# A fused attention and mixture-of-experts kernel: weight pieces split elsewhere in the opening, unused products in TensorE's waits, record scatters issued later

## The chip, the core and the metric

The kernel runs on one core of a Trainium2 chip. The metric is the device time of one execution in microseconds. Before the change three timed runs gave 1045.49, 1046.57 and 1046.40 us, median 1046.4. One further execution was profiled; its own time is 1038.92 us, and its span from first to last instruction is 1037.2 us.

## The reference

Three layers in a row over 4608 tokens (8 batches of 576), model width 512, hidden width 1024:

```python
# attention, in chunks of 64 tokens, 8 heads of 64
scores = scale * np.matmul(q_c, k_c.transpose(0, 1, 2, 4, 3))
attn = softmax(scores)
out = np.matmul(attn, v_c)                      # -> x, (4608, 512)
# first feed-forward layer
h = x @ w_in                                    # (4608, 1024)
solu = h * softmax(h)
ln = (solu - mean) / np.sqrt(var + 1e-06) * g_ln
x2 = ln @ w_out                                 # (4608, 512)
# mixture of 8 experts: one expert for each token
e_idx = np.argmax(x2 @ w_gate, axis=1)
out[mask] = gate_w[mask, None] * eom[mask, e, None] * (relu(x2[mask] @ w1[e]) @ w2[e])
```

The gain `g_ln` is a factor of each row of `w_out`, and the kernel multiplies it into the weights.

## The kernel before

The work is in units of 128 tokens, 36 of them. Every large product is made from fp32 values split in a rounded high part and a remainder (the low part), as three products: high by high, high by low weight, low by high weight. So every weight must be split too: the high part by a copy that rounds, the low part by a subtraction of source minus high part.

Each engine has its own instruction order, written out by hand as steps `s` from -2 to 35; engines wait for each other by semaphores. In step `s` unit `s` is in its first-layer products (`H_ps`, 24 products of 128x512, L458), unit `s - 1` in its second-layer products (`Y_ps`, 24 products), unit `s + 1` has its probabilities transposed (L475) and multiplied by v (`mixed`, L534 to L547), and unit `s + 2` has its scores made (`scores`, L521 to L532). "H(0)" below is the first-layer products of unit 0, "Y(0)" the second-layer products of unit 0.

The path of one unit: TensorE makes scores; VectorE takes the maximum and subtracts it (L948, L951); ScalarE takes the exponential in place (L767); VectorE sums, adds 1e-9 (L957), inverts and multiplies (L962, semaphore `norm`); TensorE transposes the result; ScalarE copies it to SBUF (`pT`, L703); TensorE multiplies by v; ScalarE makes the high part `xh` (L703), VectorE the low part `xl` (L899); then H. VectorE takes the maximum of a row of H (L922), ScalarE the exponential (L747), VectorE multiplies (L930) and subtracts the mean (L937); TensorE transposes the rows, ScalarE makes `dh`, VectorE `dl`; then Y. GpSimd makes the factor of each row (`xs_ops`), and ScalarE applies it when it copies Y out (L776).

The opening, steps -2 to 1, has another job beside this: 4 MB of first-layer weights, in 8 pieces of 128x1024. Pieces 0 to 3 are `w_in`, pieces 4 to 7 `w_out`. SyncE's queue loads a piece into one of four staging places (`HOME`); ScalarE makes its high part at the places of its program that `HIGH_PIECES` names (L716 to L728); for pieces 4 to 7 it first multiplies both halves by `g_ln`, in place. The low part is made by VectorE for pieces 1 to 3 (`LOW_PIECES`, L901 to L905), by GpSimd for 0 and 4 to 7 (L1242 to L1245). Between pieces 0 and 4 GpSimd issues nine DMAs that fill a table (L1297 to L1300). Step 0 of SyncE then loads the first expert's weights over two of the staging places, and GpSimd splits those.

Later, once in four units, the routing of four units is worked out, and GpSimd scatters their records to the table by four indirect DMAs (`send`, L1288 to L1294), as soon as VectorE has them. The second phase (the experts) begins when the last unit is through; nothing of it is touched.

## Time and profile before

| | |
|---|---|
| median of three runs | 1046.4 us |
| profiled execution, its own time | 1038.92 us |
| its span | 1037.2 us |
| TensorE busy | 1011.7 us (98%) |
| VectorE, ScalarE, GpSimd busy | 545.9, 403.0, 259.7 us |
| share of TensorE in the chain that ended last | 92% |
| 0 to 36.4 us: TensorE busy | 20.59 us |

How the rows further down are read. A row of the timeline gives start (us from the span's start), duration (us), engine, line and operation, output and input, xcount of merged instructions, and in brackets the idle time of the engine before it and what ended that. A row of the chain of waits gives start, duration and what. A row of a stretch gives its length, then busy time and count for TensorE, its weight loads, VectorE, ScalarE and GpSimd, then the granted clock, the busy share of the DMA engines and GB/s. Starts of neighbouring matmuls overlap a little, since each one's end is modelled.

### The profile page before, as it was taken

To read this page: it belongs to the slowest core of one execution; us is meant where nothing else is said; L and a number is where in the kernel's file an instruction comes from. 1 tells how busy PE (TensorE), PEld (TensorE's weight loads), DVE (VectorE), ACT (ScalarE), POOL (GpSimd) and SP (SyncE) were. 2 spreads that over 40 slices of the span, in tenths; PEclk is the share of its full clock that TensorE was granted. 3 is DMA by queue.
4 is the path that set the end of the run, shared out by engine and by line. 5 is a ranking of instruction groups with operands and counts; after the bars stand their busy time and mean duration, and the time that the engine had idled before them with its cause. 6 is when DMAs were issued, how large, how long until landed. Compare 5 with 4: busy or idle time off the path is not lost.

```text
span 1037.2 us, 24250 instructions
## 1 busy us (share of the span) xinstructions
PE 1011.7 (98%) x7323; PEld 837.9 (81%) x7324; DVE 545.9 (53%) x1137; ACT 403.0 (39%) x733; POOL 259.7 (25%) x458
## 2 busy tenths in 40 slices
PE   5899999999999999999999999999999999999997
PEld 4788888888888888888878788888888888888885
DVE  5676767677666767676737534244243332342521
ACT  5544434444334444344422533233333432342521
POOL 5772202113031312122223222122222221122211
PEclk9999999999999999999999999999999999999999
DMA  8452332322122322222013444334232331341110
GB/s 294 158 163 82 48 81 78 82 82 73 61 72 82 82 75 53 78 82 62 22 52 102 173 133 160 122 94 122 90 122 91 112 122 50 100 127 55 34 41 30
DMA packets 43024, 97.15 MB, mean 94 GB/s; under 512 B 9678, under 2 KB 9806, under 8 KB 42960
## 3 DMA queue, kind: packets, MB, share of 16 engines
q1 hardware_dynamic: 31616, 75.51, 23.6%
q0 software_dynamic: 9248, 20.70, 6.3%
q8 instruction: 46, 0.75, 0.3%
q10 hardware_dynamic: 2096, 0.04, 0.1%
q14 instruction: 18, 0.15, 0.0%
HBM read 76.66 MB, written 20.60 MB: 94 GB/s over the span
## 4 chain that ended last, share of the span: by engine, by line
PE 92%; DMA 3%; issue 1%; ACT 1%; SPq 1%; DVE 1%; POOL 0%; POOLq 0%; DVEq 0%; ACTq 0%
PE Y_ps L442 38%; PE H_ps L442 38%; PE X L434 7%; PE S L434 3%; PE S L530 2%; PE X L544 2%; DMA stage<-in_experts 1%; PE L_ps L518 1%; DMA stage<-in_moe_w_in 1%; PE L_ps L442 1%; SPq L391 0%; DMA xg<-x_rows,slot_rec 0%; POOL route_table L1293 0%; DVE dl L899 0%; ACT stage L726 0%
## 5 line engine op out<-in xcount | busy, mean ns | idle before, releaser
L442 PE MATMUL Y_ps<-wx,dh 128*128 128x512 f32 (+1 forms) x1184 | 376.3, 399 | 1.3 <-DVE dl L899 1.3
L442 PE MATMUL H_ps<-wx,xh 128*128 128x512 f32 (+1 forms) x1216 | 334.4, 397 | 2.9 <-DVE xl L899 2.3
L442 PEld LDWEIGHTS H_ps<-wx,xh 128*128 128x128 f32 x1216 | 223.4, 189 | 46.1 <-issue 2.4
L442 PEld LDWEIGHTS Y_ps<-wx,dh 128*128 128x128 f32 x1184 | 214.1, 188 | 43.9 <-DVE dl L899 1.4
L442 PE MATMUL Y_ps<-wx,dl 128*128 128x512 f32 (+1 forms) x592 | 231.8, 391 | 0.0
L442 PE MATMUL H_ps<-wx,xl 128*128 128x512 f32 (+1 forms) x608 | 187.9, 390 | 0.0
L899 DVE TENSOR_TENSOR dl<-X,dh 128x512 fp32r<-128x512 f32 x152 | 97.6, 684 | 80.8 <-ACT dh L703 80.8
L899 DVE TENSOR_TENSOR wx<-stage,wx (+1 forms) x58 | 70.5, 1225 | 122.0 <-ACT wx L865 119.4
L442 PEld LDWEIGHTS H_ps<-wx,xl 128*128 128x128 f32 x608 | 114.4, 188 | 24.5
L442 PEld LDWEIGHTS Y_ps<-wx,dl 128*128 128x128 f32 x592 | 111.1, 188 | 24.4
L922 DVE TENSOR_REDUCE nmax_h<-H_ps 128x1 f32<-128x1024 f32 x36 | 44.1, 1224 | 85.3 <-PE H_ps L442 85.3
L703 ACT ACTIVATE stage<-S 128x512 f32<-128x512 f32 x36 | 21.5, 598 | 170.9 <-PE S L434 170.9
L703 ACT ACTIVATE dh<-X 128x512 fp32r<-128x512 f32 x152 | 81.7, 592 | 7.4 <-DVE i_load L1184 4.4
L1251 POOL TENSOR_TENSOR var<-sumsq 128x1 f32<-128x1 f32 x36 | 7.0, 193 | 300.3 <-ACT stage L761 300.3
L803 ACT ACTIVATE cen<-H_ps 128x512 f32<-128x512 f32 x40 | 23.9, 597 | 145.5 <-PE H_ps L442 145.5
L434 PE MATMUL X<-ident,cen 128*128 128x128 f32 x608 | 78.8, 272 | 0.2 <-ACT cen L803 0.2
L434 PEld LDWEIGHTS X<-ident,cen 128*128 128x128 f32 x608 | 70.7, 140 | 10.2 <-ACT cen L803 0.3
L865 ACT ACTIVATE wx<-stage x56 | 58.6, 1058 | 44.7 <-issue 23.2
L1339 POOL DMA_INDIRECT out<-x,slot_rec x40 | 41.9, 1047 | 134.5 <-ACT x L829 121.9
L829 ACT ACTIVATE x<-Y_ps,slot_rec 128x512 f32<-128x512 f32 x39 | 26.8, 687 | 115.8 <-PE Y_ps L442 115.8
L1069 DVE TENSOR_SCALAR cen<-H_ps 128x512 f32<-128x512 f32 x40 | 27.6, 690 | 78.5 <-PE H_ps L442 78.5
L930 DVE SCALAR_TENSOR_TENSOR cen<-H_ps,cen 128x1024 f32<-128x1024 f32 x36 | 44.1, 1225 | 30.2 <-ACT cen L747 30.2
(199 smaller groups left out, 1026.0 us busy)
## 6 DMA issues: line engine op xcount, KB each, us to landing
stage<-in_experts SPq DMA_DIRECT2D x64, 512.0 KB, 3.5
stage<-in_q SPq DMA_DIRECT2D x36, 256.0 KB, 3.1
stage<-in_k SPq DMA_DIRECT2D x36, 256.0 KB, 3.8
stage<-in_v SPq DMA_DIRECT2D x36, 256.0 KB, 3.6
x_rows<-x SPq DMA_DIRECT2D x36, 256.0 KB, 2.0
stage<-in_moe_w_out SPq DMA_DIRECT2D x4, 512.0 KB, 5.2
stage<-in_moe_w_in SPq DMA_DIRECT2D x3, 512.0 KB, 7.1
slot_rec<-route_table POOLq DMA_DIRECT2D x40, 2.0 KB, 2.7
```

The costliest lines, as they stand in the source:

```text
L434: last = pe.transpose(to[:, i * n:(i + 1) * n], x, idn)
L442: i = pe.matmul(acc[:, c0:c0 + HALF], x[:, kk, :], w(part, kk * cols + c0), start=first and x is hi and part == 0, stop=last and x is lo)
L530: i = pe.matmul((S_ps, T0)[a][e * CH:(e + 1) * CH, r * CH:(r + 1) * CH], qT[b][rows, 2 * r + e, :], kT[b][rows, 2 * r + e, :], start=True, ...
L703: act.activation(out_, in_, ACT.Copy).then_inc(done, 1)
L803: act.activation(hs[:, 0:HALF], H_ps[:, 0:HALF], ACT.Relu).then_inc(h0_ev, 1)
L829: act.activation(yb[(u + 1) % 2][:, :], Y_ps[:, :] if has(0) else H_ps[:, 0:DM], ACT.Copy, scale=slot_rec[(u + 3) % 4][:, 2:3].bitcast(f32 ...
L865: act.activation(hi, src, ACT.Copy).then_inc(split_hi, 1)
L899: dve.tensor_tensor(out_, whole, high.bitcast(f32), ALU.subtract).then_inc(done, 1)
L922: dve.tensor_reduce(nmax_h[:, 0:1], H_ps[:, :], AX.X, ALU.max, negate=True).then_inc(hmax, 1)
L930: dve.scalar_tensor_tensor(cen[:, :], H_ps[:, :], 1.0, cen[:, :], ALU.mult, ALU.mult, accum_out=sum_t[:, 0:1]).then_inc(he_done, 1)
L1069: dve.tensor_scalar(hs[:, HALF:], H_ps[:, HALF:], 0.0, None, ALU.max).then_inc(h1_ev, 1)
L1339: pool.indirect_dma_start(out, bass.IndirectOffsetOnAxis(ap=slot_rec[(u + 3) % 4][:, 1:2].bitcast(u32), axis=0), yb[(u + 1) % 2][:, :], No ...
```

## The change

- Piece 4 gets a fifth staging place and is loaded behind the first two units' rows, without a wait. Pieces 5, 6 and 7 move to other places and wait for other pieces. Pieces 6 and 7 are issued ahead of unit 3's q and k.
- ScalarE makes the high part of piece 3 one step later, behind the copy `pT` of unit 0 (the place "prob").
- Pieces 5 and 7 are no longer scaled in place: ScalarE scales and rounds in one instruction per half, and VectorE makes the low part as source times gain minus high part, one instruction per half: piece 5 behind the maximum of H(0), piece 7 behind unit 2's subtraction.
- GpSimd makes the low part of piece 0 in two halves, the second behind `norm` of unit 0; that of piece 4 between the table's fifth and sixth DMA; that of piece 6 behind them.
- TensorE makes 20 products into `Y_ps` that nothing reads (`warm`), at six places of steps -2 to 0.
- A chunk's four scatters wait for `pv_done` of the next step, that is for the products with v of the next step.

```diff
...
 
-        staged = [x[:, :].rearrange("p (l n) -> p l n", l=2) for x in (spare, cen)] + [raw[:, b, :, :] for b in range(2)]
-        HIGH_PIECES = {(-2, "begin"): (0,), (-2, "exp"): (1, 2, 3), (-1, "x"): (4,), (-1, "exp"): (5,), (0, "x"): (6, 7)}
-        LOW_PIECES = {(-2, "norm"): (1,), (-1, "x"): (2, 3)}
+        staged = [x[:, :].rearrange("p (l n) -> p l n", l=2) for x in (spare, cen)] + [raw[:, b, :, :] for b in range(2)] + [stage[:, 0:4:3, 1, :]]
+        HIGH_PIECES = {(-2, "begin"): (0,), (-2, "exp"): (1, 2), (-1, "prob"): (3,), (-1, "x"): (4,), (-1, "exp"): (5,), (0, "x"): (6, 7)}
+        LOW_PIECES = {(-2, "norm"): (1,), (-1, "x"): (2, 3), (0, "max"): (5,), (0, "exp"): (7,)}
+        ACT_SCALED = (4, 6)
 
-        HOME = (0, 1, 2, 3, 0, 2, 3, 0)
-        USE = (0, 0, 0, 0, 1, 1, 1, 2)
+        HOME = (0, 1, 2, 3, 4, 0, 2, 3)
+        USE = (0, 0, 0, 0, 0, 1, 1, 1)
 
...
                 else:
-                    free, count = {4: (wlow_pool, 1), 5: (wlow_dve, 2), 6: (wlow_dve, 3), 7: (wlow_pool, 2)}[i]
-                    sp.wait_ge(free, count)
+                    if i > KD:
+                        sp.wait_ge(*{5: (wlow_pool, 1), 6: (wlow_dve, 2), 7: (wlow_dve, 3)}[i])
                     rows = w_out[(i - KD) * 2 * P:(i - KD + 1) * 2 * P, :]
...
             load_v(0, 1, 1)
+            load_first(KD)
             sp.wait_ge(qk_done, 1)
             load_qk(0, 2, 0)
-            for i in range(KD, KD + 2):
-                load_first(i)
+            load_first(KD + 1)
 
...
                 s = c * UN + u
-                if has(4) and not (isinstance(s, int) and s == -2):
-                    sp.wait_ge(qk_done, s + 3)
-                    load_qk(c + 1, u, u % 2)
                 if isinstance(s, int) and s == -1:
...
                         load_first(i)
+                if has(4) and not (isinstance(s, int) and s == -2):
+                    sp.wait_ge(qk_done, s + 3)
+                    load_qk(c + 1, u, u % 2)
                 if has(3) and not (isinstance(s, int) and s == -2):
...
                 if isinstance(s, int) and s == 0:
-                    sp.wait_ge(wlow_pool, 5)
+                    sp.wait_ge(wlow_pool, 3)
+                    sp.wait_ge(wlow_dve, 5)
                     for p in range(2):
...
 
+            def warm(count):
+
+                hi = first_at(0, 0)
+                for _ in range(count):
+                    pe.matmul(Y_ps[:, :], hi[:, 0, 0:P], hi[:, 1, :], start=True, stop=True)
+
             def step(c, u, has):
...
                     transposed(T1, [x2[u % 2][:, kk * P:(kk + 1) * P] for kk in range(KD)], ident[:, :]).then_inc(x2_tp, 1)
+                if isinstance(s, int) and s == 0:
+                    warm(2)
                 if has(1):
...
                     transposed(T0, [prob[:, 2 * r:2 * r + 2, :].rearrange("p a c -> p (a c)") for r in range(4)], ident[:, :]).then_inc(pt_tp, 1)
+                if isinstance(s, int) and s in (-1, 0):
+                    warm(s + 2)
                 if has(-1):
...
                     scores(c, u, b)
+                if isinstance(s, int) and s == -2:
+                    pe.wait_ge(wsplit_hi, 1)
+                    warm(6)
+                if isinstance(s, int) and s == -1:
+                    warm(3)
                 if has(1) and not (isinstance(s, int) and s == -1):
                     mixed(c, u, has)
+                if isinstance(s, int) and s == 0:
+                    warm(6)
                 if has(-1):
...
                 if isinstance(s, int) and s == 1 and kk % 2 == 0:
-                    pe.wait_ge(wlow_pool, kk // 2 + 2)
+                    low, count = ((wlow_pool, 2), (wlow_dve, 4), (wlow_pool, 3), (wlow_dve, 5))[kk // 2]
+                    pe.wait_ge(low, count)
 
...
                         f = (i - KD) * 2
-                        for l in range(2):
-                            act.activation(staged[HOME[i]][:, l, :], staged[HOME[i]][:, l, :], ACT.Copy, scale=gl[:, f + l:f + l + 1]).then_inc(wscaled, 1)
-                        act.wait_ge(wscaled, (i - KD + 1) * 2)
-                        act.activation(first_at(0, i), staged[HOME[i]], ACT.Copy).then_inc(wsplit_hi, 1)
+                        if i in ACT_SCALED:
+                            for l in range(2):
+                                act.activation(staged[HOME[i]][:, l, :], staged[HOME[i]][:, l, :], ACT.Copy, scale=gl[:, f + l:f + l + 1]).then_inc(wscaled, 1)
+                            act.wait_ge(wscaled, ACT_SCALED.index(i) * 2 + 2)
+                            act.activation(first_at(0, i), staged[HOME[i]], ACT.Copy).then_inc(wsplit_hi, 1)
+                        else:
+                            act.activation(first_at(0, i)[:, 0, :], staged[HOME[i]][:, 0, :], ACT.Copy, scale=gl[:, f:f + 1])
+                            act.activation(first_at(0, i)[:, 1, :], staged[HOME[i]][:, 1, :], ACT.Copy, scale=gl[:, f + 1:f + 2]).then_inc(wsplit_hi, 1)
 
...
                     copy(pT[:, :, :], quad(T0, H), pt_ev)
+                first_high(s, "prob")
                 if has(0):
...
                     dve.wait_ge(wsplit_hi, i + 1)
-                    less(first_at(1, i), staged[HOME[i]], first_at(0, i), wlow_dve)
+                    if i < KD:
+                        less(first_at(1, i), staged[HOME[i]], first_at(0, i), wlow_dve)
+                    else:
+                        lo, x, hi, f = first_at(1, i), staged[HOME[i]], first_at(0, i).bitcast(f32), (i - KD) * 2
+                        dve.wait_ge(gl_in, 48)
+                        dve.scalar_tensor_tensor(lo[:, 0, :], x[:, 0, :], gl[:, f:f + 1], hi[:, 0, :], ALU.mult, ALU.subtract)
+                        dve.scalar_tensor_tensor(lo[:, 1, :], x[:, 1, :], gl[:, f + 1:f + 2], hi[:, 1, :], ALU.mult, ALU.subtract).then_inc(wlow_dve, 1)
 
...
                     dve.tensor_reduce(nmax_h[:, 0:1], H_ps[:, :], AX.X, ALU.max, negate=True).then_inc(hmax, 1)
+                first_low(s, "max")
                 if has(-2):
...
                                       smax[:, :].rearrange("p (r a) -> p r a", a=2).unsqueeze(3).to_broadcast([P, H // 2, 2, CH]), ALU.subtract).then_inc(ssub, 1)
+                    first_low(s, "exp")
                     dve.wait_ge(exp_s, s + 3)
...
 
+            def first_low_half(i, l):
+
+                return pool.tensor_tensor(first_at(1, i)[:, l, :], staged[HOME[i]][:, l, :], first_at(0, i)[:, l, :].bitcast(f32), ALU.subtract)
+
             def xs_ops(s):
...
                 if u == 2 and has(-2) and not (isinstance(c, int) and c == 0):
+
+                    wait_alone(pool, pv_done, min(s + 3, NT) if isinstance(s, int) else s + 3, passed)
                     send(c)
...
 
-            first_low(0)
+            pool.wait_ge(wsplit_hi, 1)
+            first_low_half(0, 0)
+            pool.wait_ge(norm, 1)
+            first_low_half(0, 1).then_inc(wlow_pool, 1)
             for n in range(8):
+                if n == 5:
+                    first_low(KD)
                 rows = table.rearrange("(p m n) r -> m p n r", p=P, m=8)[n]
...
             pool.dma_start(x2d[0:1, :], zrow).then_inc(pads, 16)
-            for i in range(KD, PIECES):
-                first_low(i)
+            first_low(KD + 2)
+
             def gather_known(i, to, free, count):
```

In TensorE's program (S is a bank of scores or transposed probabilities, X the products with v, stage the loaded q, k and v), from the first scores to the first products of unit 0, before:

```order
L530 MATMUL S<-stage 64x64 x16
L434 MATMUL S<-ident,prob 128x128 x4
L544 MATMUL X<-stage 64x64 x16
L530 MATMUL S<-stage 64x64 x16
L442 MATMUL H_ps<-wx,xh 128x512 x4
```

And with the change:

```order
L549 MATMUL S<-stage 64x64 x16
L452 MATMUL Y_ps<-wx 128x512 x6
L436 MATMUL S<-ident,prob 128x128 x4
L452 MATMUL Y_ps<-wx 128x512
L563 MATMUL X<-stage 64x64 x16
L549 MATMUL S<-stage 64x64 x16
L452 MATMUL Y_ps<-wx 128x512 x3
L444 MATMUL H_ps<-wx,xh 128x512 x4
```

Ten of the twenty products stand ahead of H(0); the other ten stand at three places between H(0) and H(1).

In ScalarE's program (wx are the split weights, stage or cen the loaded piece, gl the gain), from the second piece of weights to the piece of step 0, before:

```order
L721 ACTIVATE wx<-cen 128x1024
L721 ACTIVATE wx<-stage 128x1024 x2
L703 ACTIVATE stage<-S 128x512
L703 ACTIVATE xh<-X 128x512
L726 ACTIVATE stage<-stage,gl 128x512 x2
L728 ACTIVATE wx<-stage 128x1024
L767 ACTIVATE prob<-prob 128x512
L726 ACTIVATE stage<-stage,gl 128x512 x2
L728 ACTIVATE wx<-stage 128x1024
L703 ACTIVATE stage<-S 128x512
```

And with the change:

```order
L741 ACTIVATE wx<-cen 128x1024
L741 ACTIVATE wx<-stage 128x1024
L723 ACTIVATE stage<-S 128x512
L741 ACTIVATE wx<-stage 128x1024
L723 ACTIVATE xh<-X 128x512
L747 ACTIVATE stage<-stage,gl 128x512 x2
L749 ACTIVATE wx<-stage 128x1024
L792 ACTIVATE prob<-prob 128x512
L751 ACTIVATE wx<-stage,gl 128x512
L752 ACTIVATE wx<-stage,gl 128x512
L723 ACTIVATE stage<-S 128x512
```

Piece 3 moved behind the copy of unit 0's transposed probabilities, and piece 5 has two half instructions where it had two and a whole one. Piece 7 in step 0 changed in the same way.

In VectorE's program, from the maximum of H(0) to unit 2's sum (cen is the row of H in work), before:

```order
L922 TENSOR_REDUCE nmax_h<-H_ps 128x1
L930 SCALAR_TENSOR_TENSOR cen,sum_t<-H_ps,cen 128x1024
L899 TENSOR_TENSOR xl<-X,xh 128x512
L934 TENSOR_SCALAR nmean<-sum_t 128x1
L935 TENSOR_SCALAR den<-sum_e 128x1
L937 TENSOR_SCALAR cen<-cen,nmean 128x1024
L940 RECIPROCAL rden<-den 128x1
L948 TENSOR_REDUCE smax<-S 128x8
L951 TENSOR_TENSOR prob<-S,smax 128x512
L955 TENSOR_REDUCE ssum<-prob 128x8
```

And with the change:

```order
L953 TENSOR_REDUCE nmax_h<-H_ps 128x1
L935 SCALAR_TENSOR_TENSOR wx<-stage,gl,wx 128x512
L936 SCALAR_TENSOR_TENSOR wx<-stage,gl,wx 128x512
L962 SCALAR_TENSOR_TENSOR cen,sum_t<-H_ps,cen 128x1024
L924 TENSOR_TENSOR xl<-X,xh 128x512
L966 TENSOR_SCALAR nmean<-sum_t 128x1
L967 TENSOR_SCALAR den<-sum_e 128x1
L969 TENSOR_SCALAR cen<-cen,nmean 128x1024
L972 RECIPROCAL rden<-den 128x1
L980 TENSOR_REDUCE smax<-S 128x8
L983 TENSOR_TENSOR prob<-S,smax 128x512
L935 SCALAR_TENSOR_TENSOR wx<-stage,gl,wx 128x512
```

Two pairs of half-piece instructions came in: one ahead of the product with the exponential, one (its first half is the last row shown) ahead of unit 2's sum.

## Rows read from the trace of the kernel before

**Rows 1.** Stretches: the opening, all up to 1000 us, and five microseconds of DMA.

```profile
0.00:36.40 36.40, 20.59 (x229) 16.35 (x230) 21.06 (x60) 22.69 (x34) 21.84 (x41) 1.00 0.75 244
36.40:1000.00 963.60, 961.55 (x6956) 797.39 (x6957) 518.80 (x1069) 373.57 (x689) 233.88 (x413) 1.00 0.30 90
10.00:15.00 5.00, 2.52 (x56) 2.12 (x60) 2.68 (x4) 2.84 (x5) 5.00 (x9) 1.00 1.05 391
```

**Rows 2.** The chain of waits, opening and step 2: start us, us, what.

```profile
16.22 7.48 PE H_ps L442 x24
...
26.63 1.33 ACT stage L726 x2
...
30.30 1.06 ACT wx L728
...
33.28 0.70 DVE ssum L955
...
35.06 1.29 DVE dl L899 x2
...
44.34 5.46 PE H_ps L442 x24
```

**Rows 3.** Timeline of TensorE in the opening.

```profile
11.67 1.11 PE L434 MATMUL S<-ident,prob 128*128 128x128 f32 x4 [4.82 <-DVE prob L962]
13.60 1.13 PE L544 MATMUL X<-stage 64*64 64x64 f32 x32 [0.81 <-ACT stage L703]
...
16.22 2.04 PE L442 MATMUL H_ps<-wx,xh 128*128 128x512 f32 x4 [0.63 <-issue]
...
28.15 1.17 PE L442 MATMUL H_ps<-wx,xh 128*128 128x512 f32 x4 [2.08 <-DVE xl L899]
...
35.19 0.66 PE L434 MATMUL S<-ident,prob 128*128 128x128 f32 x4 [0.42 <-DVE prob L962]
36.39 0.73 PE L442 MATMUL Y_ps<-wx,dh 128*128 128x512 f32 x2 [0.54 <-DVE dl L899]
```

**Rows 4.** Timeline of ScalarE in the opening: piece 3, unit 0's xh, piece 4.

```profile
12.00 1.06 ACT L721 ACTIVATE wx<-stage 128x1024 fp32r<-128x1024 f32 x1 [0.22 <-DMA stage<-in_moe_w_in]
...
14.80 0.60 ACT L703 ACTIVATE xh<-X 128x512 fp32r<-128x512 f32 x1 [1.25 <-PE X L544]
17.52 1.33 ACT L726 ACTIVATE stage<-stage,gl 128x512 f32<-128x512 f32 x2 [2.12 <-DMA stage<-in_moe_w_out]
```

**Rows 5.** Timeline of VectorE, opening and step 2; last, all 36 of L957.

```profile
9.85 0.81 DVE L957 TENSOR_SCALAR ssum<-ssum 128x8 f32<-128x8 f32 x1
...
16.03 2.35 DVE L899 TENSOR_TENSOR wx<-stage,wx 128x1024 fp32r<-128x1024 f32 x2
...
23.72 1.23 DVE L922 TENSOR_REDUCE nmax_h<-H_ps 128x1 f32<-128x1024 f32 x1 [0.29 <-PE H_ps L442]
26.21 1.23 DVE L930 SCALAR_TENSOR_TENSOR cen<-H_ps,cen 128x1024 f32<-128x1024 f32 x1 [1.27 <-ACT cen L747]
...
59.00 1.49 DVE L962 TENSOR_TENSOR prob<-prob,srec 128x512 f32<-128x512 f32 x1
...
L957 DVE TENSOR_SCALAR ssum<-ssum x36: 171/172/1249, 9.8 to 501.8; 128x8 f32<-128x8 f32 x36
```

**Rows 6.** Timeline of GpSimd: piece 0's low part, and a copy in step 2.

```profile
8.27 2.35 POOL L1245 TENSOR_TENSOR wx<-stage,wx 128x1024 fp32r<-128x1024 f32 x1 [4.30 <-ACT wx L721]
...
58.91 1.04 POOL L1238 CAST wx<-stage 128x1024 fp32r<-128x1024 f32 x1
```

**Rows 7.** One chunk's scatters (all 36: min/median/max ns), and the step beside them.

```profile
L1293 POOL DMA_INDIRECT route_table<-rec,posi x36: 954/964/1267, 120.0 to 551.7; - x36
...
125.17 0.60 ACT L703 ACTIVATE xh<-X 128x512 fp32r<-128x512 f32 x1 [1.50 <-PE X L544]
...
125.16 0.76 DVE L937 TENSOR_SCALAR cen<-cen,nmean 128x1024 f32<-128x1024 f32 x1
...
128.57 1.03 PE L434 MATMUL X<-ident,cen 128*128 128x128 f32 x8
```

More of the change, by code:

```diff
@@ L203, in build @@
         passed, zeroed, consts, gl_in, padset, pads = sems("passed zeroed consts gl_in padset pads")
-        wraw_in = [sem(f"wraw_in{i}") for i in range(4)]
+        wraw_in = [sem(f"wraw_in{i}") for i in range(5)]
         wscaled, wsplit_hi, wlow_dve, wlow_pool = sems("wscaled wsplit_hi wlow_dve wlow_pool")
@@ L362, in step @@
                 s = c * UN + u
+                if isinstance(s, int) and s == -1:
+                    for i in range(KD + 2, PIECES):
+                        load_first(i)
                 if has(4) and not (isinstance(s, int) and s == -2):
@@ L365, in step @@
                     load_qk(c + 1, u, u % 2)
-                if isinstance(s, int) and s == -1:
-                    for i in range(KD + 2, PIECES):
-                        load_first(i)
                 if has(3) and not (isinstance(s, int) and s == -2):
@@ L488, in step @@
                     scores(c, u, b)
+                if isinstance(s, int) and s == -2:
+                    pe.wait_ge(wsplit_hi, 1)
+                    warm(6)
+                if isinstance(s, int) and s == -1:
+                    warm(3)
                 if has(1) and not (isinstance(s, int) and s == -1):
                     mixed(c, u, has)
+                if isinstance(s, int) and s == 0:
+                    warm(6)
                 if has(-1):
```

## The prediction

> **What bounds the kernel now.** I read the engine shares first, then the stretches. In the opening, 0 to 36.4 us, TensorE is busy 20.59 us, so it sits idle for 15.8 us; in the 963.6 us behind it, for 2.05 us [rows 1]. From 36.4 us on TensorE sets the time, and what another engine does there costs nothing unless it makes TensorE late. So the change is worth by how much Y(0), the first products after which TensorE never stops, starts before 36.39 us [rows 3].
>
> The chain of waits tells what leads there [rows 2]: H(0) from 16.22 for 7.48 us, unit 1's path to H(1) at 28.15 [rows 3], and then not TensorE but ScalarE with pieces 6 and 7 (26.63 to 31.36), unit 2's sum at 33.28, `dl` at 35.06 to 36.35, Y(0). H(1) and the transposes inside it end at 34.77 (35.19 less its idle 0.42) [rows 3]. So there are two ways into Y(0), TensorE's and ScalarE's, and both must shorten.
>
> One more fact is in the same rows. H(0) takes 7.48 us, the same 24 products in step 2 5.46 us [rows 2]; its first four take 2.04 us, the first four of H(1) 1.17 [rows 3]. The granted clock stands at 1.00 in all the opening's stretches [rows 1], so that column does not show it, but the durations are those of the lower of TensorE's two levels (1.2 GHz), and the later ones those of 2.4 GHz. Before it TensorE had idled 4.82, 0.81 and 0.63 us between short work [rows 3].
>
> **Part 1: up to the start of H(0).** Halving piece 0's low part takes GpSimd off VectorE's way. L957 takes 0.81 us there and 0.17 as median [rows 5], beside GpSimd's subtraction at 8.27 to 10.62 [rows 6]. One half ends by 9.5, before L957 at 9.85; `norm` comes 0.64 earlier, at about 11.0. The six unused products start at about 8.25 (piece 0's high part is ready then, [rows 6]) and cost at most 0.51 each at the lower level (2.04 / 4): they end at 11.3 at the latest, more likely 11.2. The transposes start there instead of 11.67 and end at 12.3 (1.11 us); the copy takes 0.6: 12.9. The one product fits in that wait of 0.81. Products with v: 12.95 to 14.1 at the lower level (1.13), 13.6 at the upper. Piece 3's high part (1.06 us, landed by 12.0, [rows 4]) now runs beside them, 12.9 to 13.95, so `xh` starts at 14.0 to 14.1 instead of 14.80. H(0) stands 1.42 us behind `xh` (14.80 to 16.22): 15.4 to 15.5. The scores of unit 1 and the three products must be through by then: scores end at 15.0 at the lower level and the three would end at 16.5, at the upper at 14.1 and 14.8. I take 15.4: 0.8 gained.
>
> **Part 2: H(0) and unit 1.** With the clock up H(0) takes 5.46 instead of 7.48 and ends at 20.9. It can't be used whole. VectorE must finish `norm` of unit 1 ahead of the maximum of H(0); it now ends at 23.43 (23.72 less 0.29 idle, [rows 5]). It follows the low parts of pieces 2 and 3 (16.03 to 18.38), which follow `xl`, so it moves up by the 0.8 of part 1. It also holds the longest L957 (1.25 us, [rows 5]), while GpSimd makes piece 4's low part. With piece 4 loaded earlier that falls elsewhere: behind piece 3 (at most 12.0) there are 1280 KB (q, k, v of unit 1, piece 4), at 391 GB/s [rows 1] 3.4 us, so it lands at 15.4; ScalarE needs 1.33 + 1.06 = 2.4 us, and GpSimd works from 17.8 to 20.15. L957 comes at about 20.4. So 1.08 is gained: `norm` ends at 23.43 - 0.8 - 1.08 = 21.55. The maximum of H(0) starts there: 2.15 earlier, and not the 2.8 of TensorE alone. The margin of 0.25 is thin; a late piece 4 costs up to those 1.08.
>
> The two half instructions for piece 5 (128x512 each; L930 does 128x1024 in 1.23, [rows 5], so some 1.3) fill the 1.27 us in which VectorE waited for ScalarE's exponential. Piece 5's high part is due at 22.8. Its load waits for piece 0's low part (second half of 2.35 us behind `norm`: 12.2, or 13.4 behind piece 1's), then unit 2's q and k and piece 5, 1024 KB, follow piece 4: landed at 18.1; ScalarE reaches it at about 19.5. No charge. The unused products around the transposes cost 4 x 0.23 = 0.9 us (5.46 / 24 each), beside VectorE's 21.55 and ScalarE's copy; the last six 1.4 us, in the 2.08 us ahead of H(1). No charge. H(1) starts at 28.15 - 2.15 = 26.0.
>
> **Part 3: to Y(0).** TensorE: H(1) ends at 34.77 - 2.15 = 32.6, the transposes at 33.1 or 33.2. ScalarE: piece 7 loses one of its instructions, 2.39 us become 1.33, so the chain from 26.63 moves up by 2.15 + 1.06 = 3.2: unit 2's sum at 30.1, `dl` done at 33.15, both ways equal. But piece 7's low part now stands in VectorE's program ahead of that sum: piece 7's high part is done at 28.15, the pair takes 1.3, done at 29.45, which is free. Unless it is blocked: GpSimd makes piece 6's low part at the same time, from 26.9 to 29.3 (2.35 us, [rows 6]). At 59.00 an instruction with two SBUF inputs took 1.49 us [rows 5], beside GpSimd's copy from 58.91 to 59.95 [rows 6]: it waited. Then the pair ends at 30.6 and costs 0.5. I take it blocked: Y(0) at 33.65, 2.7 gained; free it would be 3.2. The Trainium skill says the same (SBUF — State Buffer, "Who interferes with whom": a VectorE instruction with two SBUF inputs contends with a GpSimd one that reads SBUF, and the second waits for the first to end). By that rule the 2.7 would stand; by the opposite reading 3.2.
>
> If the clock is up before the products with v, part 1 gains 0.3 more and `norm` with it. With half of that: **2.9 us**.
>
> **Part 4: the scatters.** TensorE is busy without a gap there. A chunk's four scatters start behind the products with v (`xh` starts at 125.17) and last 4 x (0.96 + 0.3 issue) = 5.1 us [rows 7]. `xs_ops` of that unit comes up to 3 us later; ScalarE reads its result a whole step later. Value 0. Bounds: no gain is to be had, since 2.05 us of idle time is all there is [rows 1]; the loss if they block VectorE is in rival C.
>
> **The sum.** Own time 1038.92 - 2.9 = 1036.0, span 1034.3. The median of the runs stands 7.5 us above the profiled execution, and I take the same difference off it: 1046.4 - 2.9 = **1043.5 us**. About 0.2% (2.1 us, so 1044.3) can be told from no change.
>
> **Rivals.**
> A: the clock does not rise before H(0). For it: scores, transposes and products with v from 11.67 to 15.6 did not raise it before, and the first products of H(0) were still slow. Against: six large products without a pause, and the transposes at once behind them, were not there. The three products then run at the lower level and end at 16.5, H(0) at 24.0, H(1) at 28.4, TensorE's way ends at 35.5; ScalarE's, 1.06 - 0.3 earlier, at 35.6, or 36.1 if blocked: gain 0.3 to 0.8, 1045.9 us. The Trainium skill (TensorE: Matmul & The Clock Gate, Part 1) says that the array starts at the lower level, that sustained activity lifts it, and that the moment is not tied to the kernel's start. By that rule forecast and rival could each come in different executions. A rise in the middle of H(0) gives 1044.5.
> B: VectorE or a load is late in the opening (piece 4 past 15.6, L957 blocked again): 1.08 lost of 2.9, 1044.6.
> C, the slower side: the scatters hold VectorE up. L937 starts at 125.16, just where they now begin, and TensorE wants its result at 128.57 against 125.92: 2.65 us of room [rows 7]. If VectorE were blocked for all 5.1 us, each chunk would lose 2.4, and seven chunks in the loop 17: 1060 us. It decides from 2.65 us of blocking per chunk. Against: each scatter is apart from the next by 0.3 us, in which VectorE gets on, and one takes 0.96 us, so a single block stays inside the room.
> D: the change does not do what it says, because the unused products come to stand on the path: all twenty cost at most 10 x 0.51 + 10 x 0.23 = 7.4 us, against 4.82 + 0.81 + 0.63 + 2.08 = 8.3 us of waits of before. If all fell outside, 7.4 - 2.9: 1050.9; if half, 1047.2.
>
> **Chances.** Forecast (1042.4 to 1044.3): 0.60; better than it 0.06; A whole or in part 0.18, of which a third still reads as faster; B 0.09, half of it faster; C 0.03; D 0.04, half of it slower. Faster by over 0.2%: 0.60 + 0.06 + 0.06 + 0.04 = 0.76, less 0.04 for what runs differ by: 0.72. Slower by over 0.2%: 0.03 + 0.02 = 0.05. Within: 0.23. The range reaches from 1042.0 (3.2 with nothing blocked, 0.3 more with the clock up early, and 0.9 for the median, since three runs lay 1.1 us apart) to 1046.0 (A whole).
>
> **What would show it.** Right: first products of H(0) at 1.17 us for four; L957 0.17 at units 0 and 1; maximum of H(0) at 21.5 directly behind `norm`; H(1) at 26.0; Y(0) at 33 to 33.7; no new idle time of TensorE after it. Wrong: 2.04 us for the first four (A); ScalarE waiting for a piece of `w_out` behind 15.6 (B); transposes of `cen` late once in four units (C); unused products directly ahead of a product that was already released (D).

## The result, and the profile after

The changed kernel takes 1035.04 us (median of 5 runs, 1034.9 to 1035.17), the kernel before 1046.4 us beside it (5 runs, 1045.49 to 1047.85): ratio 0.989, 95% interval 0.988 to 0.9901. That is faster, by 11.4 us; 2.9 were forecast, and the range ended at 1042.0. The traced execution of the changed kernel lasted 1035.17 us with a span of 1033.6. For before these were 1038.92 and 1037.2. So the traces differ by 3.75 us, the medians by 11.4: the greater part of the gain is in no row of either trace.

TensorE's timeline in the opening after the change, in the order of [rows 3] (start us, us, engine, line, operation, count, idle before it and what ended it):

```profile
8.28 2.93 PE L452 MATMUL Y_ps<-wx 128*128 128x512 f32 x6 [1.69 <-ACT wx L741]
11.01 1.06 PE L436 MATMUL S<-ident,prob 128*128 128x128 f32 x4
11.71 0.78 PE L452 MATMUL Y_ps<-wx 128*128 128x512 f32 x1
12.75 1.13 PE L563 MATMUL X<-stage 64*64 64x64 f32 x32 [0.26 <-ACT stage L723]
...
15.37 1.17 PE L444 MATMUL H_ps<-wx,xh 128*128 128x512 f32 x4
...
25.82 1.16 PE L444 MATMUL H_ps<-wx,xh 128*128 128x512 f32 x4 [0.17 <-issue]
...
33.74 0.73 PE L444 MATMUL Y_ps<-wx,dh 128*128 128x512 f32 x2 [0.54 <-DVE dl L924]
```

The first four products of H(0) take 1.17 us and not 2.04, so the clock is at the upper level there; all 24 take 5.59 us. H(0) starts at 15.37, H(1) at 25.82, Y(0) at 33.74, against 16.22, 28.15 and 36.39. VectorE in the same stretch, against [rows 5]:

```profile
9.59 0.17 DVE L990 TENSOR_SCALAR ssum<-ssum 128x8 f32<-128x8 f32 x1
...
20.27 0.17 DVE L990 TENSOR_SCALAR ssum<-ssum 128x8 f32<-128x8 f32 x1
...
21.32 1.22 DVE L953 TENSOR_REDUCE nmax_h<-H_ps 128x1 f32<-128x1024 f32 x1
22.46 0.74 DVE L935 SCALAR_TENSOR_TENSOR wx<-stage,gl,wx 128x512 fp32r<-128x512 f32 x1
...
28.29 1.77 DVE L935 SCALAR_TENSOR_TENSOR wx<-stage,gl,wx 128x512 fp32r<-128x512 f32 x1 [0.34 <-ACT wx L752]
29.98 0.74 DVE L936 SCALAR_TENSOR_TENSOR wx<-stage,gl,wx 128x512 fp32r<-128x512 f32 x1
```

Both long L957 (now L990) are gone. The half instruction of piece 7 (28.29) takes 1.77 us where the same one of piece 5 takes 0.74: GpSimd makes piece 6's low part beside it, from 27.11 for 2.40 us:

```profile
27.11 2.40 POOL L1278 TENSOR_TENSOR wx<-stage,wx 128x1024 fp32r<-128x1024 f32 x1 [4.77 <-ACT wx L749]
```

Behind Y(0) nothing has changed that these two traces can show (stretches as in [rows 1]):

```profile
0.00:33.70 33.70, 25.21 (x248) 19.43 (x249) 22.86 (x64) 20.56 (x32) 18.47 (x40) 1.00 0.80 269
33.74:1000.00 966.26, 964.82 (x6972) 800.37 (x6973) 519.65 (x1071) 374.53 (x690) 232.43 (x414) 1.00 0.28 90
```

TensorE is idle there for 1.44 us (966.26 less 964.82), against 2.05 in [rows 1]. So the opening gives 2.65 us, the rest of the traces 0.95 (1033.6 - 33.74 = 999.86 against 1037.2 - 36.39 = 1000.81), and some 7.6 us of the medians' 11.4 are left to be found.

### The profile page after: what moved, and what is told of

It reads as the page before. It is cut to its first block, busy times and chain, and to the rows that moved or that the text cites. A ratio compares the mean times of both kernels' runs of the same rounds, so it can differ in the third digit from the quotient of the medians.

```text
span 1033.6 us, 24309 instructions
## 1 busy us (share of the span) xinstructions
PE 1016.0 (98%) x7343; PEld 841.0 (81%) x7344; DVE 547.3 (53%) x1141; ACT 400.9 (39%) x731; POOL 253.9 (25%) x457
## 4 chain that ended last, share of the span: by engine, by line
PE 94%; DVE 2%; issue 1%; ACT 1%; DMA 1%; ACTq 0%; POOLq 0%; DVEq 0%; SPq 0%
PE Y_ps L444 39%; PE H_ps L444 39%; PE X L436 8%; PE S L436 3%; PE S L549 2%; PE X L563 2%; PE L_ps L537 1%; PE L_ps L444 1%; DMA stage<-in_moe_w_in 1%; DVE dl L924 0%; PE Y_ps L452 0%; ACT stage L747 0%; ACT dh L723 0%; ACT stage L723 0%; POOLq L64 0%
## 5 line engine op out<-in xcount | busy, mean ns | idle before, releaser
L1383 POOL DMA_INDIRECT out<-x,slot_rec x40 | 41.9, 1047 | 137.6 <-ACT x L854 126.1
L1332 POOL DMA_INDIRECT route_table<-rec,posi x36 | 39.0, 1082 | 96.9 <-PE X L563 61.6
```

Source lines behind the costliest of these rows:

```text
L1332: pool.indirect_dma_start(table, bass.IndirectOffsetOnAxis(ap=posi[:, u:u + 1], axis=0), rec[:, u, :], None).then_inc(rec_st, 16)
L1383: pool.indirect_dma_start(out, bass.IndirectOffsetOnAxis(ap=slot_rec[(u + 3) % 4][:, 1:2].bitcast(u32), axis=0), yb[(u + 1) % 2][:, :], No ...
```

## The experiments

Each comparison ran on one chip, with the kernel before beside it. It took 1038.33 us on chip 1, 1047.15 on chip 8, 1038.66 on chip 12, 1047.27 on chip 7 and 1038.8 on chip 9: two groups of chips, about 8.6 us apart. Chips are named only by these numbers.

### The two parts apart, chip 1

The kernel before again, with no edit:

> The kernel before, unchanged, for the trace of one more execution: the first one lasted 1038.92 us, the timed runs 1046.4. Theory S (something that the scatters set off costs 7.5 us, and was absent in the first traced execution): a trace of 1046 us has TensorE idle, or slower products, once in four units from step 6 on. Theory O (the opening costs them): TensorE's idle time before Y(0) is 7.5 us longer than the 15.8 us of before. Theory T (the end of the kernel, the last output scatters): the extra time stands behind the last product.

1039.17 us (10 runs, 1038.11 to 1040.04); traced, 1038.11, Y(0) at 36.40. On this chip it takes 1038, so its trace is once more not of a kernel that takes 1046.

The wait of the scatters alone, put into the kernel before:

```
+                    wait_alone(pool, pv_done, min(s + 3, NT) if isinstance(s, int) else s + 3, passed)
                     send(c)
```

> Kernel before with the scatter part of the change alone (each chunk's four scatters wait for the products with v of the next step). Theory S: 1046.4 - 8.7 = 1037.7 us, the change's 11.4 less the 2.65 that the opening's trace shows. Theories O and T: 1046.4, no difference. My prediction had valued this part at 0.

1038.17 us, ratio 1.0006 to before: nothing on this chip.

The changed kernel without that line:

> Changed kernel without the scatter part, so the opening's part alone. Theory S: 1046.4 - 2.65 = 1043.7 us. Theory O: 1035.0, the whole of the change. Theory T: either, since the end is the same in both.

1035.12 us (6 runs, 1034.91 to 1035.44), ratio 0.9967 (0.9955 to 0.998): 3.2 us faster, and that is the time of the whole change.

The changed kernel without its unused products (all five calls of `warm` taken out):

> Changed kernel without its twenty unused products. By the prediction H(0) then starts at the lower level of TensorE's clock: 7.48 us instead of 5.46, Y(0) at 33.7 + 0.6 to 1.5 = 34.3 to 35.2, so 1035.6 to 1036.5 us. Rival: the products did nothing for the path, since VectorE's norm of unit 1 held the maximum of H(0) anyway: 1035.0, and Y(0) at 33.7.

1038.44 us (10 runs, 1036.13 to 1039.44), ratio 0.9994: in the median all of the opening's gain goes with them, more than the 1035.6 to 1036.5 that were expected. The runs differ by their granted clock: the one at 0.999 took 1036.13 us, the four at 0.995 took 1039.03 to 1039.44. So where the clock stays up in the waits some 2 us of the gain stand without the unused products; e6_holdonly below says the same. The trace (1039.38 us), TensorE at H(1):

```profile
27.82 2.05 PE L444 MATMUL H_ps<-wx,xh 128*128 128x512 f32 x4 [2.10 <-DVE xl L913]
```

H(0) ran at the lower level (8.01 us for 24), as in rival A, and H(1) started at the lower level again, after the wait of 2.10 us for `xl`; the granted clock over 0 to 42 us is 0.92. Y(0) starts at 37.43. The kernel before does the same in part of its executions (f0_before, below).

### The opening's pieces, chip 8

The changed kernel with no edit:

> The changed kernel, unchanged, beside the kernel before, once more. In the first comparison it took 1035.04 and the kernel before 1046.4; in the comparison after it the kernel before took 1038.33 in 27 runs. Theory C (some 8 us of the first comparison are not of the change, but of that comparison's runs of the kernel before): 1035.0 against 1038.3, gain 3.3. Theory R (the kernel before has an extra cost that comes and goes and which the change takes away): some comparison shows 1046 again, and with the changed kernel never.

1035.14 us (4 runs) against 1047.15: ratio 0.9887 (0.987 to 0.9903). The 12 us appear on this chip, with the changed kernel as fast as on chip 1.

Without the last six unused products, ahead of H(1):

```
-                if isinstance(s, int) and s == 0:
-                    warm(6)
```

> Changed kernel without the last six unused products, those ahead of H(1). Without any of the twenty the trace showed H(1) at TensorE's lower level from 27.82 on, after a wait of 2.10 us. Theory K (the six keep the clock up through that wait): executions spread, some at 1035.0, some up to 2.7 us longer, median 1035.0 to 1036.5. Rival (the earlier ones are enough, since the wait is now after more work at the upper level): 1035.0 with a spread under 0.6 us.

1035.32 us (4 runs, to 1035.86). Its trace is of the longest of them, TensorE at H(1):

```profile
25.79 2.05 PE L444 MATMUL H_ps<-wx,xh 128*128 128x512 f32 x4 [1.76 <-DVE xl L922]
```

There the clock fell in a wait of 1.76 us, and Y(0) came at 34.12. The execution took 1035.86, the three others 1035.28 to 1035.33: the fall came in one of four here, and cost about 0.5 us. The spread of 0.58 us is that of the rival, but the fall is that of theory K.

With the last six alone (the other four calls of `warm` out):

> Changed kernel with the last six unused products alone. H(0) starts at the lower level (7.5 to 8.0 us instead of 5.6), H(1) at 27.8 instead of 25.8, Y(0) at 35.7: 1036.5 to 1037.0 us, and by theory K without the executions at 1039.4 that none of the twenty gave.

1036.44 us, 1.3 more than the changed kernel. H(1) is at 27.51 at the upper level, Y(0) at 35.09. So the early unused products are worth 1.3 us, and the last six save what the clock's fall would cost in a wait of 2.1 us (1038.44 less 1036.44, across two chips).

ScalarE's high part of piece 7 ahead of piece 6's (shown in part; VectorE's and GpSimd's wait counts for the two pieces change with it):

```
-(0, "x"): (6, 7)}
+(0, "x"): (7, 6)}
```

> Changed kernel in which ScalarE makes the high part of piece 7 ahead of that of piece 6. In the changed kernel's trace the first half of piece 7's low part takes 1.77 us on VectorE and the second 0.74, beside GpSimd's low part of piece 6 (27.11 to 29.51), and unit 2's sum starts behind them at 30.64. Theory B (that is the port's block of 1.0 us, and 0.5 us of it is on the path to Y(0)): both halves take 0.74, the sum starts at 30.1, Y(0) at 33.2, 1034.5 us. Rival (TensorE's own way, H(1) and the transposes, holds Y(0) anyway): 1035.0.

1035.65 us, 0.5 slower than the changed kernel, and neither of the two times expected. VectorE, then GpSimd:

```profile
27.80 0.74 DVE L935 SCALAR_TENSOR_TENSOR wx<-stage,gl,wx 128x512 fp32r<-128x512 f32 x1
28.46 2.88 DVE L936 SCALAR_TENSOR_TENSOR wx<-stage,gl,wx 128x512 fp32r<-128x512 f32 x1
...
28.27 2.52 POOL L1278 TENSOR_TENSOR wx<-stage,wx 128x1024 fp32r<-128x1024 f32 x1 [5.82 <-ACT wx L749]
```

The first half now runs free, but GpSimd's low part of piece 6 starts at 28.27, near its end, and the second half takes 2.88 us. The block is moved, not removed.

### Once more apart, with a better version, chip 12

The kernel before, its scatters' wait alone, and the opening alone, as on chip 1:

> The kernel before, unchanged, for a trace: the same kernel takes 1038.3 us (27 runs) on one chip and 1047.2 (7 runs) on another, the changed one 1035.0 to 1035.1 on both. If this runs where it takes 1047: theory S puts 7.5 to 9 us into steps with scatters (some 1 us in each of eight, TensorE idle or stretched there); theory O into the first 40 us; theory T behind 1000 us. Where it takes 1038 nothing is decided.

> Kernel before with the scatter part alone. On a chip where the kernel before takes 1047: theory S 1038.2 (as on the other chip), theories O and T 1047. On a chip where it takes 1038: 1038.2 by all.

> Changed kernel without the scatter part. On a chip where the kernel before takes 1047: theory S 1035.1 + 9 = 1044, theory O 1035.1, theory T 1044 or 1035. On a chip where it takes 1038: 1035.1 by all.

1039.18, 1038.48 and 1035.21 us against 1038.66: the same as on chip 1, so no part can be told guilty here. The trace of f0_before (1039.85 us) shows H(1) at the lower level behind the wait:

```profile
28.52 2.05 PE L442 MATMUL H_ps<-wx,xh 128*128 128x512 f32 x4 [2.09 <-DVE xl L899]
```

Executions of the kernel before lie between 1037.8 and 1041.2 us here, all those above 1039 with a granted clock of 0.994 to 0.996, and those of the opening alone between 1035.05 and 1035.37.

The changed kernel with GpSimd's low part of piece 6 cut in two, the second half behind unit 2's `norm`, away from VectorE's pair:

```
-            first_low(KD + 2)
+            pool.wait_ge(wsplit_hi, KD + 3)
+            first_low_half(KD + 2, 0)
+            pool.wait_ge(norm, 3)
+            first_low_half(KD + 2, 1).then_inc(wlow_pool, 1)
```

> Changed kernel with GpSimd's low part of piece 6 in two halves, the second behind norm of unit 2. With the high parts swapped, VectorE's second half instruction for piece 7 took 2.88 us, because GpSimd's 2.4 us began between the two; so the port's block decides, and the swap only moved it. Theory B: the first GpSimd half runs 27.1 to 28.4, VectorE's pair takes 0.74 each, the sum starts at 30.1, Y(0) at 33.2: 1034.6 us. Rival (TensorE's own way holds Y(0)): 1035.0.

1034.71 us (6 runs, 1034.53 to 1035.11), ratio 0.9959 (0.9946 to 0.9971). VectorE and then TensorE at Y(0):

```profile
28.10 0.75 DVE L935 SCALAR_TENSOR_TENSOR wx<-stage,gl,wx 128x512 fp32r<-128x512 f32 x1 [0.34 <-ACT wx L752]
28.77 0.75 DVE L936 SCALAR_TENSOR_TENSOR wx<-stage,gl,wx 128x512 fp32r<-128x512 f32 x1
29.99 0.69 DVE L988 TENSOR_REDUCE ssum<-prob 128x8 f32<-128x512 f32 x1 [0.48 <-ACT prob L792]
```

```profile
33.10 0.73 PE L444 MATMUL Y_ps<-wx,dh 128*128 128x512 f32 x2 [0.45 <-DVE dl L924]
```

Both halves take 0.75 us, and Y(0) starts 0.64 earlier than 33.74. Of that 0.19 lies ahead of H(1) (25.63 against 25.82), so 0.45 is what the block had cost. This is the fastest version that was run; against the changed kernel it is compared across chips only (1034.71 against 1035.04 and 1035.14).

### Where the other 8 us were, chip 7

The same three kernels on a chip where the kernel before takes 1047 us:

> The kernel before, unchanged, as one of the compared kernels, so that it also leaves a trace on the chip of this comparison. If the chip is one on which it takes about 1046 to 1047 us, its trace should show where the extra 8 to 9 us lie against the execution of 1038.9 us: theory S (scatters) puts them at the record scatters, between 120 and 135 us; theory O (opening) before Y(0), so Y(0) would begin at about 44 us and not at 36.4; theory T (tail) spreads them over the stretch from 140 us to the end, at the same granted clock. If the chip is one on which it takes 1038 to 1039 us, nothing of the three is told apart.

> The kernel before with the wait of the record scatters alone. On a chip where the kernel before takes about 1047: theory S gives 1038 to 1039, theory O gives 1047, theory T gives 1047. On a chip where it takes 1038 to 1039: 1038.5 by all.

> The changed kernel without the wait of the record scatters, so the opening alone. On a chip where the kernel before takes about 1047: theory S gives 1043.5 to 1044, theory O gives 1035, theory T 1043.5 to 1044. On a chip where it takes 1038 to 1039: 1035.2 by all.

Before, unchanged, 1047.35 us (9 runs); with the scatters' wait alone 1038.16 (3 runs, 1037.95 to 1038.18; ratio 0.9917, 0.9898 to 0.9937); with the opening alone 1043.47 (6 runs, 1043.32 to 1043.55; ratio 0.9965, 0.9952 to 0.9978). This is what theory S (the scatters) gave, within 0.03 us; theories O and T gave 1047 for the wait alone. And g0_before is the first trace of the kernel before at such a time (1048.18 us). TensorE there, at the third unit of the first set:

```profile
125.70 0.69 PE L530 MATMUL S<-stage 64*64 64x64 f32 x32
126.22 0.39 PE L544 MATMUL X<-stage 64*64 64x64 f32 x10
127.55 0.61 PE L544 MATMUL X<-stage 64*64 64x64 f32 x22 [0.93 <-issue]
128.09 0.72 PE L442 MATMUL Y_ps<-wx,dh 128*128 128x512 f32 x2
```

The same place of e0_before, on chip 1:

```profile
123.94 0.69 PE L530 MATMUL S<-stage 64*64 64x64 f32 x32
124.45 0.65 PE L544 MATMUL X<-stage 64*64 64x64 f32 x32
125.03 0.50 PE L442 MATMUL Y_ps<-wx,dh 128*128 128x512 f32 x1
```

In g0_before TensorE stops for 0.93 us inside one run of 32 small products, which have no wait between them; "issue" says that the profile knows of nothing it waited for. GpSimd is at its fourth scatter:

```profile
121.82 1.12 POOL L1293 DMA_INDIRECT route_table<-rec,posi  x1 [4.26 <-DVE id_out L1044]
123.25 0.99 POOL L1293 DMA_INDIRECT route_table<-rec,posi  x1 [0.31 <-issue]
124.54 0.96 POOL L1293 DMA_INDIRECT route_table<-rec,posi  x1 [0.30 <-issue]
125.81 0.96 POOL L1293 DMA_INDIRECT route_table<-rec,posi  x1 [0.30 <-issue]
```

All of TensorE's idle time of this kind from 100 to 500 us in g0_before (us in total, times, longest):

```profile
PE X L544 <- issue: 5.9, 7, 0.9
```

and in g2_opening, which has the opening but not the wait (its L563 is L544 of before; one of its seven stalls is in two pieces):

```profile
PE X L563 <- issue: 5.8, 8, 1.0
```

In g1_scatter, e0_before and the trace of before this view is empty in the stretch, and in g0_before and g2_opening it shows no more stalls up to 1000 us. So the stall comes once in each of seven sets of scatters. What one costs is more than its 0.8 us of idle time. The second set's first scatter starts at 180.28 in g0_before and the third's at 238.75, 58.47 apart; in e0_before these are 177.20 and 234.47, 57.27 apart. That is 1.20 us a set, 8.4 us for seven. With the opening's 3.3 it makes 11.7, between the 11.4 and 12.0 measured for the whole change. The traces agree: from Y(0) to the end g0_before takes 1008.2 us (1046.4 - 38.21) and e0_before 999.9 (1036.3 - 36.40), 8.3 apart. The two gains measured on chip 7 itself, 9.1 and 3.8, add up to 12.9. They can't simply be added: the three runs with the wait alone all had a granted clock of 0.999, those of the kernel before 0.994 to 0.998, so part of the 9.1 is the clock's fall at H(1) and not the stalls.

### What TensorE waits for there, chip 9

The profile has a DMA queue of kind "instruction", q8, which brings one packet of 16 KB at a time (0.75 MB in 46 packets over the execution). Its packet next to the stall, in windows of 0.2 us (queue, packets, MB, share of 16 engines' time in the window): of g0_before from 127.80 us, and behind it of g1_scatter from 125.40 us.

```profile
q8 instruction: 1, 0.02, 94.8%
```

```profile
q8 instruction: 1, 0.02, 29.1%
```

94.8% of 16 x 0.2 us are 3.03 us for one packet beside the scatters, 29.1% are 0.93 us where they wait. In e0_before, on the chip without the stall, it is 2.59 us, so a long packet alone doesn't make the stall. The packet starts 0.25 us or more behind TensorE's going on at 127.55. I took the place for a sign of a refill of TensorE's instructions, and three kernels were to test it.

Sixteen products of the scores repeated in the first unit of each set (8 units):

```
-                for r in range(H // 2):
+                for r in [0] * (16 // len(TILES)) * (u == 0) + list(range(H // 2)):
```

> The kernel before with the first four products of the scores repeated four times more in the first unit of each set (16 products, 32 records, in 8 units), far from the scatters: TensorE's stream of instructions is longer there, the order and the scatters' distance to the products of the third unit are as before. Added cost 8 x about 0.55 us, some 4.5 us. Only on a chip where the kernel before takes about 1047 us do the theories differ. Theory R (TensorE's instruction refill meets the scatters; the idle of 0.8 us stands at a fixed place of the stream): the idle moves by about 32 records to the front, into the scores or their end, or goes away where it no longer meets a scatter. Theory W (the small products themselves, or their operands, are held by the scatters): it stays after 9 to 11 of the 32 products with v. Time by both 1050 to 1052 while the idle is there, 1043 to 1044 if it goes away.

The scatters waiting for the scores (the added line with `qk_done` for `pv_done`), and only the fourth waiting for the products with v:

> The kernel before, its record scatters waiting for the scores of the third unit (the products right ahead of those with v), not for those with v: the first scatter begins about 1.2 us behind the scores, so about where the products with v end, the others behind. If the idle needs a scatter under way in the products with v: the time is 1038 to 1039 on every chip. If a scatter just ahead or just behind is enough, about 1047 on a chip where the kernel before takes 1047.

> The kernel before, only the fourth record scatter of each set waiting for the products with v; the first three start where they start before, some 1.7 us ahead of that unit's last products. On a chip where the kernel before takes about 1047: if the idle comes from the last scatter, the one beside the products with v, 1038 to 1039; if it comes from what the first three leave in the queues, still 1047. On a chip where it takes 1038 to 1039: 1038.5 by both.

```
+                    if u == UN - 1 and s is not None:
+                        wait_alone(pool, pv_done, min(s + 3, NT) if isinstance(s, int) else s + 3, passed)
                     pool.indirect_dma_start(...
```

On this chip the kernel before takes 1038.8 us, so the stall did not occur and the main questions were not answered: 1043.18, 1038.52 and 1038.67 us. One thing h1_shift did show. The packet that starts in the 0.2 us from 125.2 in e0_before starts in those from 122.2 in h1_shift, though the work itself stands 1.4 us later (first scatter at 121.44 against 120.03), and here it takes 0.96 us:

```profile
q8 instruction: 1, 0.02, 30.0%
```

The whole execution has 49 packets of q8 in place of 46. Only TensorE's stream was made longer, and the packets went with it: q8 brings TensorE's instructions. The Trainium skill (Runtime: NRT & Kernel Launch, "Instruction fetch mechanics") says that an engine fetches instructions over a DMA queue of its own, in blocks of 16 KiB, and calls the cost of crossing a block mostly hidden. The packets' size agrees.

The stall is not this refill, and the trace of g0_before shows it. A refill would need a packet at each of the seven stalls. The third and the fifth stall:

```profile
243.25 0.34 PE L544 MATMUL X<-stage 64*64 64x64 f32 x9
244.43 0.63 PE L544 MATMUL X<-stage 64*64 64x64 f32 x23 [0.84 <-issue]
...
360.16 0.39 PE L544 MATMUL X<-stage 64*64 64x64 f32 x10
361.35 0.61 PE L544 MATMUL X<-stage 64*64 64x64 f32 x22 [0.80 <-issue]
```

All DMA queues with a packet that starts from 235 to 250 us, and behind it from 357.5 to 366.5:

```profile
q1 hardware_dynamic: 538, 0.99, 29.3%
q0 software_dynamic: 128, 0.01, 0.9%
...
q1 hardware_dynamic: 392, 0.73, 42.5%
q0 software_dynamic: 98, 0.01, 1.1%
```

No instruction packet of any queue is there, and yet TensorE stops as long as at the others and at the same place, behind 9 to 11 of the 32 products. Where the blocks of the stream fall moves from set to set; the stall doesn't. That is what theory W of h1_shift's expectation says (the products or their operands are held beside the scatters).

What does stand at the same distance in each set is the fourth scatter, queue q0. Its 32 packets start at 244.1 to 244.4 in the third set, with TensorE going on at 244.43; in the fifth at 361.0 to 361.3, with 361.35. Over all seven stalls of g0_before and all seven of g2_opening, TensorE goes on 0.2 to 0.35 us behind the first of these packets. In e0_before the products with v of the first set are through at 125.03, and the packets start only at 125.5: there TensorE doesn't wait for them. This is a place in time, not yet a cause: scatters and products run in step with each other in any case.

What stays open: what holds TensorE in the stall, since no row names it and theory W was not tested by a run of its own. Which of the four scatters does it, and why chip 7 has it and 1, 9 and 12 have not, isn't known. Chip 8, and the chip of the first result, left no trace of the kernel before at 1046 or 1047 us; that theirs is the same stall rests on the sums.

## Why the prediction was wrong

**What bounds the kernel: right for the traced execution alone.** The change was taken to be worth what Y(0) comes earlier and nothing else. That left out what the timed executions had behind Y(0) and this trace had not.

**Part 1, part 2: right.** H(0) was predicted at 15.4 and came at 15.37, at the upper level. `norm` and the maximum of H(0) at 21.55, came at 21.32; H(0) 5.46 us, came 5.59; H(1) at 26.0, came at 25.82. L957 is 0.17 at both units. Rival A stayed out, and e3_nowarm shows that it is what happens without the unused products. Two margins were thinner than this reads. Piece 5 was said to land at 18.1; ScalarE waited for it until 20.15, still ahead of the 22.8 at which it was due. And in other traces of the opening the second L957 (L990) was held up again, 0.40 us in e2_opening and 0.77 in e8_half.

**Part 3: right.** Y(0) at 33.65 with the pair blocked, came at 33.74. The block was priced at 0.5 and is 0.45 by e8_half, where both halves take 0.75 us. The rule of the Trainium skill that was cited there (SBUF — State Buffer, "Who interferes with whom": the second of two instructions waits for the first to end) holds: the instruction that began at 28.29, beside GpSimd's from 27.11 to 29.51, took 1.77 us against 0.74. For the opening 2.9 us were taken; the trace gives 2.65 and the medians on chips 1 and 12 3.2 and 3.45. One part of the difference was in the text, at half its size: in e2_opening, e4_after and f2_opening the clock is up before the products with v (0.69 or 0.70 us for 32, against 1.13 in the trace of the result), and H(0) starts at 14.85 to 15.11. Another part was not in the sum: the last six unused products also keep the clock from falling in the wait ahead of H(1), which in the kernel before costs up to 2 us in some executions (1040 against 1038). I had counted them as worth nothing.

**Rival B** cost nothing, though its sign as worded came: ScalarE waited 0.63 us for piece 5 up to 20.15, behind 15.6. **Rival D** came in small: the six unused products ended at about 11.0, and the transposes behind them were released at about 10.8 (`norm` ended at 10.72, and in e3_nowarm the transposes start 0.06 us behind it). That is 0.2 us. **Rival C** had the danger on the wrong side. It asked whether the scatters in their new place hold up VectorE; no trace shows them holding it up there. In their old place, on chip 7, they held up TensorE.

**Part 4 failed.** It set the scatters at 0, with the bound that no gain is to be had, since TensorE is idle for only 2.05 us in the whole stretch. That is true of the traced execution, and on chips 1 and 12 the scatters' wait is worth 0. On chip 7 it is worth 9.1 us, 8.4 of them stalls, which I could only have allowed for if I had asked whether that trace was of the executions that were timed.

**The sum failed for the same reason.** "The median of the runs stands 7.5 us above the profiled execution, and I take the same difference off it": the difference was taken for a constant that no edit touches. It was 0.7% of the time, in runs that agree within 1.1 us, and so a cost in the kernel of those executions: on chip 7 seven stalls of 1.2 us, and for the chip of the result the same by the sums. The changed kernel's traced execution and its median differ by 0.13 us. The range had no room for it, since its lower end added only 0.9 for the median.

## What to carry to other kernels

Where the timed runs agree among themselves and the traced execution lies well outside them, the trace is of another case, and the gap is a cost that may go or stay: keep both ends, gap gone and gap kept, in the range. An edit that moves many small DMAs away from a burst of short instructions may be what removes it, as here, even where the trace shows no idle time. Before a stall is put down to a transfer, look for the transfer at every one of the stalls, not at the first. In this opening unused products were worth as much for holding the clock in a wait of 2 us as for raising it.

## What the runs showed of the hardware

- The same kernel takes 1038.3 to 1038.8 us on three chips and 1047.2 or 1047.3 on two. At the same granted clock of 0.998 its executions took 1046.2 to 1046.7 us on chip 7 and 1037.9 to 1039.4 on chips 1 and 12. So the difference is stalls of TensorE beside scatters, not the clock. The changed kernel took 1035.0 to 1035.6 on chip 8.
- On chip 7 TensorE stopped in each of seven bursts of 32 small products beside four scatters, for 0.79 to 0.93 us, with no wait in the program there. Two of the seven had no packet of instructions within 3 us.
- A packet of 16 KB in the instruction queue took 0.88 to 1.69 us at most places and 1.93 to 3.05 us at some of those beside the scatters (g0_before and e0_before). Loads of q, k and v move there too, so which of them slows it isn't shown.
- TensorE's clock fell from 2.4 to 1.2 GHz in a wait of 2.1 us (e3_nowarm, f0_before, g0_before, h3_fourth), and once in one of 1.76 us (e5_nohold); e0_before had the same wait of 2.1 us and kept the upper level. It is a matter of the execution, not of the wait's length alone.
- Two consecutive VectorE instructions, both with two SBUF inputs, 0.74 us each when free: a GpSimd instruction of 2.52 us that started near the end of the first held up the second, which took 2.88 us (e7_swap).
